# First decayed keys on VectorE, second mask ahead of the third r, and group numbers ahead of their waits in an attention and mixture-of-experts kernel

## The reference, cut to what matters

```python
for t in range(S):                                             # attention
    cur = np.einsum('bhd,bhe->bhde', u[None] * kt, vt)
    y[:, :, t] = np.einsum('bhd,bhde->bhe', rt, state + cur)
    state = w[None, :, :, None] * state + np.einsum('bhd,bhe->bhde', kt, vt)
...
do_compute = (x @ w_skip) > 0                                  # last layer
xc = x[do_compute]
e_idx = np.argmax(xc @ w_gate, axis=1)                         # gate_w: softmax of it at e_idx
for e in range(E):
    mask = e_idx == e
    y[mask] = gate_w[mask, None] * (np.maximum(xc[mask] @ w1[e], 0.0) @ w2[e])
out[do_compute] = xc + y
```

## Time and profile before

| | us |
|---|---|
| median of 3 runs | 303.61 (303.21 to 307.46) |
| the profiled execution | 303.3 |
| its span in the trace | 301.5 |
| busy in the span: PE / PEld / DVE / ACT / POOL | 290.6 / 241.3 / 182.5 / 85.8 / 63.9 |
| PE in the chain that ended last | 82% |

### The profile page before, as it was taken

The page is one execution under the profiler, slowest core; times in us unless marked ns, Lnnn a source line. Parts: engine busy times, 40 slices in busy tenths (PEclk is TensorE's granted clock), DMA queues, the critical chain, the costliest instruction groups (busy, mean ns, idle before and its releaser), DMA issues.

```text
span 301.5 us, 8498 instructions
## 1 busy us (share of the span) xinstructions
PE 290.6 (96%) x3074; PEld 241.3 (80%) x3075; DVE 182.5 (61%) x422; ACT 85.8 (28%) x181; POOL 63.9 (21%) x103
## 2 busy tenths in 40 slices
PE   7998999999999999999899999999999999999994
PEld 7977788787878887643446878899999999999994
DVE  4699979888798897447532786243262432534323
ACT  1122223132322223513221775231322313223120
POOL 1497545555546320200000010000000000000000
PEclk9999999999999999999999999999999999999999
DMA  6999898888869969999999569902020020200202
GB/s 172 273 252 284 261 280 233 255 251 258 232 207 297 269 202 400 400 430 421 426 354 364 182 228 380 335 3 104 0 104 0 0 104 0 104 0 0 104 0 104
DMA packets 31311, 62.37 MB, mean 207 GB/s; under 512 B 4912, under 2 KB 22960, under 8 KB 30256
## 3 DMA queue, kind: packets, MB, share of 16 engines
q1 hardware_dynamic: 27824, 56.70, 56.5%
q10 hardware_dynamic: 3456, 5.25, 6.3%
HBM read 52.49 MB, written 9.44 MB: 205 GB/s over the span
## 4 chain that ended last, share of the span: by engine, by line
PE 82%; DVE 5%; DMA 5%; SPq 3%; issue 2%; DVEq 1%; ACT 1%; ACTq 0%
PE ps L1530 11%; PE ps L1531 10%; PE ps L1532 10%; PE ps L1257 8%; PE ps L1199 7%; PE ps L1280 4%; PE ps L1219 4%; PE ps L1408 4%; PE ps L1427 4%; PE ps L1541 3%; PE ps L1288 3%; DMA w2e<-w2b 3%; PE ps L1269 3%; PE ps L1233 2%; DMA raw<-rT 2%
## 5 line engine op out<-in xcount | busy, mean ns | idle before, releaser
L917 DVE SCALAR_TENSOR_TENSOR h_lo<-ps,h_hi 128x512 fp32r<-128x512 f32 x48 | 32.7, 690 | 65.7 <-ACT h_hi L1108 63.1
L1530 PE MATMUL ps<-w_hi,h_hi 128*128 128x384 f32 x192 | 65.3, 340 | 1.4 <-DVE h_lo L917 0.6
L1531 PE MATMUL ps<-w_lo,h_hi 128*128 128x384 f32 x192 | 64.5, 336 | 0.0
L1532 PE MATMUL ps<-w_hi,h_lo 128*128 128x384 f32 x192 | 64.3, 335 | 0.0
L1108 ACT ACTIVATE h_hi<-ps 128x512 fp32r<-128x512 f32 x48 | 28.2, 599 | 81.0 <-PE ps L1541 75.0
L608 POOL TENSOR_TENSOR kt<-raw,dec_k 128x512 f32<-128x512 f32 x23 | 36.3, 1580 | 38.7 <-PE ps L1199 25.2
L1530 PEld LDWEIGHTS ps<-w_hi,h_hi 128*128 128x128 f32 x192 | 36.0, 188 | 5.4 <-issue 3.4
L1531 PEld LDWEIGHTS ps<-w_lo,h_hi 128*128 128x128 f32 x192 | 36.0, 188 | 1.2
L1532 PEld LDWEIGHTS ps<-w_hi,h_lo 128*128 128x128 f32 x192 | 36.0, 188 | 0.0
L738 DVE TENSOR_TENSOR at<-ps,mask 128x1024 f32<-128x1024 f32 x24 | 29.2, 1218 | 1.2 <-PE ps L1199 1.2
L992 ACT ACTIVATE xt<-ps 128x384 f32<-128x384 f32 x24 | 11.7, 491 | 61.3 <-PE ps L1288 43.3
(11 more groups left out here) (188 smaller groups left out, 376.3 us busy)
## 6 DMA issues: line engine op xcount, KB each, us to landing
w_first<-w1a SPq DMA_DIRECT2D x8, 768.0 KB, 7.4
w_first<-w2a SPq DMA_DIRECT2D x8, 768.0 KB, 7.1
a_slot<-w1a SPq DMA_DIRECT2D x4, 1536.0 KB, 15.0
x_slot<-w2a SPq DMA_DIRECT2D x3, 1536.0 KB, 13.8
out<-x SPq DMA_DIRECT2D x1, 4608.0 KB, 14.8
out<-x SPq DMA_DIRECT2D x24, 192.0 KB, 1.9
kn<-k_nat SPq DMA_DIRECT2D x20, 192.0 KB, 5.5
vn<-v_nat SPq DMA_DIRECT2D x20, 192.0 KB, 6.1
```

The source lines that it names most:

```text
L917: dve.scalar_tensor_tensor(out=h_lo[f % HB][:], in0=bank[4 + f % HB], scalar=0.0, in1=h_hi[f % HB][:].bitcast(F32), op0=ALU.max, op1=ALU.s ...
L1530: pe.matmul(bank[t][:, 0:DM], hh, w2_hi[:, f, :], start=(f == 0), stop=False)
L1531: pe.matmul(bank[t][:, 0:DM], hh, w2_lo[:, f, :], start=False, stop=False)
L1532: last = pe.matmul(bank[t][:, 0:DM], hl, w2_hi[:, f, :], start=False, stop=(f == FT - 1))
```

## The change

VectorE makes `kt(0)`, `kt(1)` and `kt(2)`, and GpSimd starts with `kt(3)`, for which it now waits until the first three are counted. In VectorE's step 1 `at(1)` is made ahead of `rt(2)`, then come `rt(2)` and `kt(2)`. Of the idle matmuls, 2 stand behind the scores of step 0 and 2 behind those of step 1, where 8 stood behind those of step 0. In the routed layer VectorE's `go_on` moves behind `low_of_h(3)` and `low_of_h(4)`, and the numbers that `group` works out for waits and addresses are named in front of the waits, on VectorE and on SP. The pieces below stand in the file's order: SP's `group`, GpSimd's steps, VectorE's steps and its `group`, TensorE's step.

```diff
-    RL_REP, KEEP = 12, 8
+    RL_REP, KEEP, KT_FIRST = 12, (2, 2), 3
...
             def group(e, g, ng, ne):
                 waits = [fixed(GT * ng + GT + t + 1) for t in range(GT)]
+                tiles = [sp.snap(g * GT + t, min_val=0, max_val=TILES - 1) for t in range(GT)]
                 go_on(sp, g_at, more, e, g)
                 for t in range(GT):
                     sp.wait_ge(y_added, waits[t])
-                    sp.dma_start(outv[:, bass.ds(g * GT + t, 1), :], x2[:, bass.ds(g * GT + t, 1), :]).then_inc(stored, 16)
+                    sp.dma_start(outv[:, bass.ds(tiles[t], 1), :], x2[:, bass.ds(tiles[t], 1), :]).then_inc(stored, 16)
...
             def step(c, b):
                 n = c * B + b
-                if n + 1 < NCHUNK * B:
+                if KT_FIRST <= n + 1 < NCHUNK * B:
                     decayed_k(n + 1)
...
                 pool.wait_ge(raw_in[b], 64 * (c + 1))
+                if n == KT_FIRST:
+                    pool.wait_ge(kt_ready, KT_FIRST)
...
+            def first_keys(n):
+
+                if n >= 2:
+                    dve.wait_ge(sc_done, n - 1)
+                dve.tensor_tensor(kt[n % 2][:], k_raw[n], dec_k[:], ALU.mult).then_inc(kt_ready, 1)
...
-                if n + 1 < NCHUNK * B:
+                if n + 1 < NCHUNK * B and n != 1:
                     decayed_r(n + 1)
                 if n == 0:
+                    first_keys(1)
                     dve.wait_ge(masks, 4)
...
                 dve.tensor_tensor(at[i][:], scores.rearrange("p (h c) -> p h c", c=C), bcast(mask[:], 1, H), ALU.mult).then_inc(at_ready, 1)
+                if n == 1:
+                    decayed_r(2)
+                    first_keys(2)
...
             decayed_r(0)
-            dve.tensor_tensor(kt[0][:], k_raw[0], dec_k[:], ALU.mult).then_inc(kt_ready, 1)
+            first_keys(0)
...
             def group(e, g, ng, ne):
+                low_of_h(3, ng)
+                low_of_h(4, ng)
                 go_on(dve, g_at, more, e, g)
-                for f in range(3, FT):
+                stored_then = dve.snap(ng * (16 * GT) + 16)
+                whole = [dve.snap(ng * GT + (t + 1 + GT)) for t in range(GT)]
+                row_at = [dve.snap((g * GT + t) * DM, min_val=0, max_val=(TILES - 1) * DM) for t in range(GT)]
+                gate_at = [dve.snap((g * GT + t) * E + e, min_val=0, max_val=TILES * E - 1) for t in range(GT)]
+                for f in range(5, FT):
                     low_of_h(f, ng)
...
-                dve.wait_ge(stored, ng * (16 * GT) + 16)
+                dve.wait_ge(stored, stored_then)
                 for t in range(GT):
-                    dve.wait_ge(y2_done, ng * GT + (t + 1 + GT))
...
+                    dve.wait_ge(y2_done, whole[t])
...
-                if one is None:
-                    keep_warm(KEEP, YT)
+                if c * B + b < len(KEEP):
+                    keep_warm(KEEP[c * B + b], YT)
```

More of the change, by code:

```diff
@@ L960, in group @@
                 dve.wait_ge(gate_ready, 1)
-                dve.wait_ge(stored, ng * (16 * GT) + 16)
+                dve.wait_ge(stored, stored_then)
                 for t in range(GT):
-                    dve.wait_ge(y2_done, ng * GT + (t + 1 + GT))
-                    row = x2[:, bass.ds(g * GT + t, 1), :].squeeze(1)
-                    dve.scalar_tensor_tensor(out=row, in0=bank[t][:, 0:DM], scalar=gate[:, bass.ds(g * GT + t, 1), bass.ds(e, 1)].squeeze(2),
+                    dve.wait_ge(y2_done, whole[t])
+                    row = x2[:].rearrange("p u d -> p (u d)")[:, bass.ds(row_at[t], DM)]
+                    dve.scalar_tensor_tensor(out=row, in0=bank[t][:, 0:DM], scalar=gate[:].rearrange("p u e -> p (u e)")[:, bass.ds(gate_at[t], 1)],
                                              in1=row, op0=ALU.mult, op1=ALU.add).then_inc(y_added, 1)
```

## The result

| | us | ratio to the kernel before |
|---|---|---|
| forecast | 302.7 (301.9 to 303.8) | |
| changed kernel, 23 runs | 305.88 median (303.01 to 312.02) | 1.0039 [1.0021, 1.0058] |
| kernel before, 23 runs beside them | 304.49 median (303.16 to 310.54) | |
| the profiled execution of the changed kernel | 312.02, span 310.3 | |

The change makes the kernel slower by 0.4%, some 1.2 us, where I forecast 0.6 us less. In the class of 2% it is "no change"; the time lies 2.1 us above my range. Two things are to be known before the rows are read. The profiled execution is the slowest of the 23, so four more of the same text (e1, e14 to e16) stand beside it where a size matters. And the kernel before has a median of 303.86 to 304.63 in the five later series, not the 303.3 that I summed against.

A forecast was written before the change was run, and what follows sets the result against it. TensorE, busy 290.6 of 301.5 us, was taken as the bound. From 303.3 us, go_on took off 0.56, the attention start and named numbers 0, giving 302.7 us, range 301.9 to 303.8.

The forecast's parts named there:

- The base: Whole kernel: summed against the profiled 303.3 us, where a median of undisturbed runs should lie; runs differ by some 0.4 us.
- The passes: Start of attention: with fewer idle matmuls, TensorE starts the scores of step 1 at 11.9 in place of 12.23 us.
- Rival 5: Start of attention: emptied TensorE stretch makes the clock fall to half rate, 2.5 to 4.5 us lost, 306.2 us; chance 0.05.
- The argument against it: Against the clock falling at the start of attention: TensorE kept full clock across the waits at 16.00 and 25.63 us.
- The keys and the mask: Start of attention, VectorE: added keys delay the first mask 0.16 us; scores of step 2 at 15.7, 0.3 us gained.
- rival 3: Attention, step 2: `kt(2)` stands behind GpSimd's `ks(1)`, scores 0.65 us later than before, 303.4 us; chance 0.10.
- the end of the argument: Attention, step 4: `rt(4)` still ends at 22.39 behind GpSimd's `kt(4)`, so the 0.3 us gain goes into a wait; counted 0.
- The mechanism: First routed group: block 3 no longer waits for `go_on`, gaining 0.86 us; slow loads behind block 4, 303 ns in later groups.
- The give-back: First routed group: block 5 behind `go_on` makes TensorE 0.38 us late, costing about 0.3 us; net gain 0.56 us.
- The named numbers: Routed layer's `group`: naming numbers ahead of waits does not reach VectorE's program and adds no SP row; counted 0.
- rival 4: Routed layer: `go_on` makes block 5 late in all groups, 0.3 us in each of 5, 304.1 us; chance 0.05.

The follow-up runs named there:

- e1: Changed kernel, text unchanged, run again for 12 timed runs and one profile: median 305.08 us, 1.0014 of the kernel before.
- e14: Changed kernel, text unchanged, one more profiled execution: 306.12 us.
- e16: Changed kernel, text unchanged, one more profiled execution: 307.07 us.
- e3: Kernel before with only the idle matmuls changed, 2 behind each of the first two scores in place of 8 behind the first: 306.13 us, 1.0043.
- the 16 runs: Of the changed kernel's 35 timed runs, text unchanged, those with a mean granted clock of 0.977 to 0.989: mean 306.8 us.
- e15: Changed kernel, text unchanged, one more profiled execution: 304.11 us.
- e8: Kernel before with only VectorE making the keys of steps 0 to 2 and masking step 1 ahead of the third r: 304.52 us, 1.0021.
- e4: Kernel before with only VectorE's go_on moved behind blocks 3 and 4 of h_lo: 303.42 us, 0.9971.
- e5: Changed kernel with no idle matmuls behind any scores: 304.08 us, 0.9976 of the kernel before.
- e2: Changed kernel with 8 idle matmuls behind the scores of step 0 and none behind step 1: 304.18 us, 0.9981 of the kernel before.

## Why the prediction was wrong, point by point

- **The base.** I summed against one execution of 303.3 us and wrote that a median of undisturbed runs should lie at it, with 0.4 us of spread. The kernel before has medians of 303.86 to 304.63 and a standard deviation of 1.3 us. This alone puts "no change" at the upper end of my range or beyond it. Three runs, one of them at 307.46, did not carry a spread of 0.4.
- **The passes: the step that failed.** I costed the smaller `KEEP` as TensorE's own time: 12 rows less, so the scores of step 1 at 11.9. That much came: they start 2.65 us behind the scores of step 0 in three of the five executions (forecast 2.75, before 3.08), and 2.86 and 3.28 in the two in which the added `kt(1)` holds `at(0)` (L748) back. But it is worth nothing by step 2, which waits for `kt(2)` and so for its tile: in e3, the passes alone, the scores of step 2 stand 6.87 us behind those of step 0, before 6.85. And the emptied row, which I priced at nothing, leaves a wait of 0.85 to 1.48 us, behind which the clock fell in two of five executions; e3 alone costs 1.0043. Rival 5 named this place and its sign. Its chance of 0.05 was the error. Its 306.2 beside the 306.8 measured in the 16 runs is luck: it counted 3.5 us on a base that was too low, and they lie 1.4 to 2.2 us above the others. The argument against it, that the clock had survived waits of 0.52 us at full grant, was drawn from waits a third to two thirds as long.
- **What no rival had.** Taking 8 matmuls and their 8 weight loads away moved TensorE's later instructions against the 16 KB pieces of q8; the wait for the late piece, 1.06 to 2.15 us in three of the five executions, is the other part of the loss. I counted what the passes took and never asked where the rest of the program comes to stand.
- **The keys and the mask.** The hold by GpSimd's `ks(1)` came as in rival 3 in three of the five executions of the changed text: `rt(2)` 1.18 and 1.33 us, `kt(2)` 1.49 us in e1. In e15 and e16 `ks(1)` began later and held `rk(1)` behind them (1.48 and 1.49 us), so `kt(2)` took 0.69 and the scores of step 2 came at 16.2. I gave the hold 0.10. The Trainium skill's rule ("SBUF — State Buffer", section "Who interferes with whom") was right, and by it I should have asked for the chance that two operations of 0.69 us miss one of 1.0 us that starts within them. The scores of step 2 did not come at 15.7 but at 16.2 to 17.0 even at full clock; part of this is a later start, since the scores of step 0 stood at 9.56 to 9.73 there, not at 9.15. And the end of the argument was wrong in the other direction: nothing of a gain was to be left at step 4, yet the waits at 25 to 31 us shrink or vanish, since GpSimd is ahead by the `kt(2)` that it did not make. By the traces loss and gain are about equal; by time e8, keys alone, has 1.0021 [0.9982, 1.0060], which is too wide to say more.
- **`go_on`.** The mechanism held: block 3 right behind its input, slow loads behind block 4, 0.30 us in later groups. The give-back was mis-sized. Block 5 started 3.11 us behind block 4's start, where I had 3.13; but I set the time at which TensorE wants its result at the start of the last L1541, and it is wanted only behind that, with 0.12 us of lateness and not 0.38. The gain is 0.86; the 0.2 us that come back do so ahead of the next group, 0.12 of them here.
- **The named numbers.** Nothing, as forecast: e4, which leaves them out, has the same 0.86 us.
- **A sum.** In rival 4, 0.3 us in each of 5 groups is 1.5 us, not 1.4; nothing hangs on it.

By the terms: group -0.65, keys about 0, low clock +0.5 to +1.0 in the mean, the moved instructions a wait of 1.06 to 2.15 us in three of the five executions of the changed text, with half rate behind each of them. The last two overlap, since half rate behind such a wait lowers the mean clock too. The sum is an estimate, some +0.5 to +1.5 us; measured are 0.4 (e1) and 1.2 us (the first 23). How the loss divides between the clock at step 1 and the late piece stays open.

## What to carry to other kernels

Idle matmuls that stand under a wait cost nothing to keep here and were no saving to remove; before taking instructions out of an engine that fetches a long program, look whether its row shows waits for "issue", and try the same edit with the count of instructions restored. If work is moved to an engine because it looks free, look at what the relieved engine will start at that moment, and whether the two exclude each other. And take the base of a sum from many runs: an effect of 0.6 us is smaller than half the standard deviation of a single one.

## What the runs showed of the hardware

- TensorE can stand still for 0.5 to 2.2 us with all inputs there, in the middle of a row of equal matmuls, until a 16 KB piece of instructions has come on q8, with the other DMA queues full (93% from 60 to 65.1 us in e1). A piece holds 256 rows of its queue and starts only once the boundary before has been passed; over the first 14 pieces of 20 traces no row behind a boundary ran sooner than 1.23 us after its piece had landed. In this kernel the wait at 65 to 72 us hangs on 8 matmuls and their 8 weight loads more or less some 50 us ahead.
- Behind the four such waits of 1.06 to 2.15 us the granted clock went to 1.2 GHz for 3.4 us; behind the eight of 0.54 to 0.79 us it did not.
- A stretch at half rate can be free: 3.41 us of it in e5 cost nothing at the scores of step 2, since TensorE was not the bound there; the same length in e2, from 18.65, came with scores of step 3 that were 1.3 us later than in e8.
